# Attention of the last two batches inside the first MLP's first quads, on three PSUM banks, with two weight slots

## What is computed

```python
mask = np.abs(pos[:, None] - pos[None, :]) < factor        # factor = 4
out = sm_attn(q_d, k_d, v_d) repeated 4 times + masked attention of q, k, v
...
h = x @ w_in                   # 512 -> 2048
x = (h - np.tanh(h)) @ w_out   # 2048 -> 512
...
gate = 1.0 / (1.0 + np.exp(-(x @ w_gate)))   # 512 -> 1536
x = (gate * (x @ w_val)) @ w_out             # 1536 -> 512
```

## Time and profile before

| | us |
|---|---|
| median of 3 runs | 949.58 (945.84 to 951.64) |
| profiled execution | 949.2 |
| its span, first to last instruction | 947.1 |
| TensorE busy in the span | 901.8 (95%) |
| VectorE, ScalarE, GpSimd busy | 577.1, 387.3, 300.5 |

### The profile page before, as it was taken

The page is one execution under the profiler, slowest core; times in us unless marked ns, Lnnn a source line. Parts: engine busy times, 40 slices in busy tenths (PEclk is TensorE's granted clock), DMA queues, the critical chain, the costliest instruction groups (busy, mean ns, idle before and its releaser), DMA issues.

```text
span 947.1 us, 15642 instructions
## 1 busy us (share of the span) xinstructions
PE 901.8 (95%) x6056; PEld 844.4 (89%) x6056; DVE 577.1 (61%) x901; ACT 387.3 (41%) x750; POOL 300.5 (32%) x251
## 2 busy tenths in 40 slices
PE   7877787999999999999998999999999999999997
PEld 5766577989999999999998999999999999999996
DVE  8777745666876566866668555556544456544445
ACT  4765645443533234433334544444322234222221
POOL 5978677674102000111015555741200001000000
PEclk8898969999999999999999999999999999999999
DMA  9677628667746464645421567679775555575411
GB/s 259 170 217 218 168 77 306 222 237 261 275 153 227 147 228 151 221 158 211 165 92 45 217 262 279 274 292 365 282 285 208 217 214 214 212 279 201 199 45 67
DMA packets 46089, 197.01 MB, mean 208 GB/s; under 512 B 3936, under 2 KB 15552, under 8 KB 33216
## 3 DMA queue, kind: packets, MB, share of 16 engines
q1 hardware_dynamic: 41984, 166.66, 48.9%
q0 software_dynamic: 4032, 29.36, 8.3%
HBM read 139.90 MB, written 56.10 MB: 207 GB/s over the span
## 4 chain that ended last, share of the span: by engine, by line
PE 79%; POOL 9%; DVE 3%; DMA 3%; issue 3%; ACT 2%; SPq 0%; POOLq 0%; DVEq 0%; ACTq 0%
PE banks L787 43%; PE banks L855 18%; PE banks L971 16%; DMA v_four<-in_v_dram 2%; POOL v_four L554 1%; POOL win L595 1%; POOL prob L561 1%; POOL mid L601 1%; POOL v_down L558 1%; ACT win L1035 1%; PE banks L765 1%; DMA qk<-in_k_dram 1%; POOL prob_d L561 1%; DVE x_op L1297 1%; PE banks L742 0%
## 5 line engine op out<-in xcount | busy, mean ns | idle before, releaser
L787 PE MATMUL banks<-x_op,pair 128*128 128x384 f32 x1512 | 278.5, 336 | 1.7 <-DVE cg_sum L1457 1.7
L787 PEld LDWEIGHTS banks<-x_op,pair 128*128 128x128 f32 x1512 | 266.7, 189 | 9.7 <-DVE cg_sum L1457 2.1
L855 PE MATMUL banks<-g_parts,mid 128*128 128x384 f32 x1152 | 228.4, 337 | 7.3 <-DVE x_all L1377 5.3
L855 PEld LDWEIGHTS banks<-g_parts,mid 128*128 128x128 f32 x1152 | 203.0, 189 | 10.2 <-DVE x_all L1377 7.3
L787 PE MATMUL banks<-x_op,win 128*128 128x384 f32 x1008 | 206.7, 342 | 4.3 <-ACT c_sum L1071 4.3
L787 PEld LDWEIGHTS banks<-x_op,win 128*128 128x128 f32 x1008 | 182.3, 193 | 5.5 <-ACT c_sum L1071 3.8
L971 PE MATMUL banks<-wout,p_parts 128*128 128x512 f32 x648 | 163.6, 393 | 1.7 <-issue 1.7
L1377 DVE TENSOR_TENSOR x_all<-banks,x_all 128x384 f32<-128x384 f32 x168 | 93.0, 555 | 83.3 <-PE banks L855 82.9
L971 PEld LDWEIGHTS banks<-wout,p_parts 128*128 128x128 f32 x648 | 120.3, 188 | 22.6 <-issue 2.1
L1482 DVE TENSOR_TENSOR x_all<-banks,x_all 128x512 f32<-128x512 f32 x90 | 62.1, 690 | 113.4 <-PE banks L971 113.4
L617 POOL DMA_DIRECT2D wout<-kept_out x12 | 6.4, 537 | 211.4 <-PE banks L971 211.4
(11 more groups left out here) (93 smaller groups left out, 1008.8 us busy)
## 6 DMA issues: line engine op xcount, KB each, us to landing
pair<-kept_pair SPq DMA_DIRECT2D x24, 1792.0 KB, 10.8
win<-kept_in SPq DMA_DIRECT2D x16, 1792.0 KB, 7.4
kept_pair<-pair SPq DMA_DIRECT2D x12, 1792.0 KB, 11.8
mid<-kept_mid POOLq DMA_DIRECT2D x16, 1024.0 KB, 5.1
kept_in<-win SPq DMA_DIRECT2D x7, 1792.0 KB, 6.8
wout<-kept_out POOLq DMA_DIRECT2D x12, 1024.0 KB, 11.7
kept_mid<-mid SPq DMA_DIRECT2D x7, 1024.0 KB, 7.0
kept_out<-wout SPq DMA_DIRECT2D x6, 1024.0 KB, 14.6
```

The source lines that it names most:

```text
L787: mm = pe.matmul(bk[:, 0:T], weights[:, w, p - 1, kk, :], x_op[:, p - 1, x, kk, :], start=(first and kk == 0 and a == 0), stop=(last and k ...
L855: mm = pe.matmul(bk[:, 0:T], w[:, wp, f, m * P:(m + 1) * P], g[:, gp, 2 * f + t, :], start=(f == 0 and a == 0), stop=(f == 1 and a == 2))
```

## The change

Only units 0 to 9 (`SOLO`) are scored in the attention's own loop, and only units 0 to 7 (`EARLY`, those which the first 768 tokens need) pass it whole. Quad 0 follows unit 7. In quad n from 1 on, unit n+9 is scored (n up to 6), one head at a time in bank 3 (`head_scores`, `head_down_scores`); unit n+8 is normalised and turned in bank 4 (n up to 7); unit n+7 is multiplied with v in two parts in bank 5 (`first_values`, `second_values`, n up to 8). Those three banks were the second set of sums, so quads 0 to 8 all use banks 0 to 2: the first product of a quad now waits until all four g tiles of the quad before it are made. The weight slots of quads 0 to 7 go from three to two, for both weights, in the space that the attention's buffers leave; the third slot is used from quad 8 on. Raw weights of quad n+1 are asked for when the products of quad n-1 are done; their sums, high and low parts are made inside quad n. Quad 0 has another order of products and splits its x in halves. The raw w_out of the second MLP's first quad is loaded earlier. The core of the diff:

```diff
+FIRST_ORDER = (1, 2, 7, 6, 5, 4, 3)
+FIRST_SPLITS = ((1, None), (2, None), (5, None), (7, 0), (6, 0), (7, 1), (4, 0), (3, 0), (6, 1), (4, 1), (3, 1))
...
+    EARLY = PAIRS * -(-SUPER // S)
+    SOLO = EARLY + 2
...
-        MID = RING + 3 * WIN_BYTES
-        G = MID + 3 * MID_BYTES
+        MID = RING + 2 * WIN_BYTES
+        G = MID + 2 * MID_BYTES
...
+        MIXED = Q1 + 1
+        def sum_banks(n):
+            return B_SUM[n % 2 if n >= MIXED else 0]
...
+                if n >= 2:
+                    sp.wait_ge(s_p1, 7 * (n - 1))
+                    sp.wait_ge(s_kept[n % 2], kept_count(n - 2))
...
+            first_t1()
+            first_t2(0)
+            first_t4(0)
+            denominators(EARLY)
+            normalise(EARLY)
+            first_t2(1)
+            first_t4(1)
+            value_sums(EARLY)
             weight_low(1)
-            weight_sums(2)
...
-                    weight_sums(n + 2)
-                    weight_low(n + 2)
+            for n in range(1, N1):
+                t = EARLY + n
+                if t < UNITS:
+                    denominators(t)
+                    normalise(t)
                 if n + 1 < Q1:
-                    plain_low(n + 1)
-                if n % Q1 == 3:
+                    weight_sums(n + 1)
+                if 1 <= n - 1 < Q1:
+                    plain_low(n - 1)
+                if n + 1 < Q1:
+                    weight_low(n + 1)
+                if t < UNITS:
+                    value_sums(t)
+                if 4 <= n < 7:
...
+            def head_scores(u, hh):
+                slot, bk, head = ring3(u), bank[B_S], slice(hh * D, hh * D + D)
+                q_u, k_u = qk[slot][:, 0, :], qk[slot][:, 1, :]
+                if hh == 0:
+                    pe.wait_ge(s_qk[slot], 32 * uses(u, ring3))
+                    pe.wait_ge(s_exd, 4 * u)
+                else:
+                    pe.wait_ge(s_sub, scored(u, 0))
+                pe.matmul(bk[:, 0:HEAD], ident_b[:, :], mask_b[:, :, :].rearrange("p n c -> p (n c)"), start=True, stop=False,
+                          skip_group_check=True)
+                for w in range(NW):
+                    rows, col = slice(w % 2 * QW, w % 2 * QW + QW), w // 2 * KW
+                    mm = pe.matmul(bk[rows, col:col + KW], q_u[head, w * QW:(w + 1) * QW], k_u[head, FIRST_KEY[w]:FIRST_KEY[w] + KW],
+                                   start=False, stop=True, skip_group_check=True)
+                mm.then_inc(s_sl, 1)
+            def head_down_scores(u, hh):
...
-                    elif n == 1:
-                        pe.wait_ge(s_cr, 2 * UNITS)
+                        pe.wait_ge(s_sub, SOLO)
+                    elif n < MIXED:
+                        pe.wait_ge(s_g, 4 * n)
+                    elif n == MIXED:
+                        pe.wait_ge(s_x, valued(UNITS - 1))
                     else:
...
             def first_quad(n):
+                u, t, v = EARLY + n + 1, EARLY + n, EARLY + n - 1
+                if v < UNITS:
+                    first_values(v)
+                if u < UNITS:
+                    head_scores(u, 0)
                 first_product(n, 1)
                 next_block(n - 2, 4)
                 first_product(n, 7)
                 next_block(n - 2, 5)
+                if v < UNITS:
+                    second_values(v)
                 first_product(n, 6)
+                if u < UNITS:
+                    head_scores(u, 1)
                 next_block(n - 2, 6)
+                if t < UNITS:
+                    turn_local(t, 0)
                 first_product(n, 2)
                 next_block(n - 2, 7)
+                if t < UNITS:
+                    turn_rest(t, 0)
                 first_product(n, 5)
+                if u < UNITS:
+                    head_down_scores(u, 0)
                 next_block(n - 1, 0)
+                if t < UNITS:
+                    turn_local(t, 1)
                 first_product(n, 4)
                 next_block(n - 1, 1)
+                if t < UNITS:
+                    turn_rest(t, 1)
                 first_product(n, 3)
+                if u < UNITS:
+                    head_down_scores(u, 1)
                 next_block(n - 1, 2)
                 next_block(n - 1, 3)
...
+            values(EARLY - 1)
+            first_product(0, 1)
+            first_product(0, 2)
+            first_product(0, 7)
+            turn_local(EARLY, 0)
+            turn_local(EARLY, 1)
+            first_product(0, 6)
+            first_product(0, 5)
+            turn_rest(EARLY, 0)
+            turn_rest(EARLY, 1)
             first_product(0, 4)
             first_product(0, 3)
             for n in range(1, N1):
...
+            def head_exps(u, hh):
+                act.wait_ge(s_mxd, scored(u, hh))
+                act.wait_ge(s_exd, 4 * u)
+                act.activation(neg_max[0:HALF, 2 * hh:2 * hh + 2], row_max[0:HALF, 2 * (SLOTS + hh):2 * (SLOTS + hh) + 2], ACT.Copy,
+                               scale=-SCALE / FACTOR ** 2).then_inc(s_neg, 1)
+                if hh == 0:
+                    act.wait_ge(s_tr, 2 * (before(u, ring3) + 1))
+                    act.wait_ge(s_den, u)
+                act.wait_ge(s_neg, scored(u, hh))
+                for a in range(2):
+                    i = 2 * hh + a
+                    col = 2 * SLOTS + i
+                    act.activation(prob_d[ring3(u)][:, i, :], bank[B_S][0:HALF, a * SD:(a + 1) * SD], ACT.Exp, bias=neg_max[0:HALF, i:i + 1],
+                                   scale=SCALE / FACTOR ** 2, accum_out=row_sum[0:HALF, col:col + 1]).then_inc(s_exd, 1)
             def copy_local(u, hh):
...
                 last, s = n % Q1 == Q1 - 1, n // Q1 + 1
-                first = n % Q1 == 0 and n > 0
-                if n > 0:
-                    g_high(n - 1, 1)
-                if skip < 1:
-                    copy_c(n, C11)
+                first = n % Q1 == 0
+                u, t, v = EARLY + n + 1, EARLY + n, EARLY + n - 1
+                if v < UNITS:
+                    copy_down(v)
+                g_high(n - 1, 1)
+                copy_c(n, C11)
                 if last:
                     x_high(s, 1)
                 if first:
                     x_high(s - 1, 4)
-                if skip < 2:
-                    copy_c(n, C22)
+                if 1 <= n - 1 < Q1:
+                    plain_high(n - 1)
+                copy_c(n, C22)
                 if last:
                     x_high(s, 7)
                 if first:
...
                 copy_c(n, C21)
                 if last:
                     x_high(s, 6)
-                if 3 <= n + 2 < Q1:
-                    weight_high(n + 2)
+                if n + 1 < Q1:
+                    weight_high(n + 1)
+                if u < UNITS:
+                    exp_local(u)
+                if t < UNITS:
+                    copy_local(t, 0)
                 tanh(n, C11)
                 if last:
                     x_high(s, 2)
+                if t < UNITS:
+                    copy_rest(t, 0)
                 tanh(n, C22)
+                if u < UNITS:
+                    head_exps(u, 0)
                 g_high(n, 0)
                 if last:
                     x_high(s, 5)
+                if t < UNITS:
+                    copy_local(t, 1)
                 tanh(n, C21)
+                if t < UNITS:
+                    copy_rest(t, 1)
                 tanh(n, C12)
-                if n == 0:
-                    weight_high(2)
-                if n + 1 < Q1:
-                    plain_high(n + 1)
+                if u < UNITS:
+                    head_exps(u, 1)
                 if n == N1 - 1:
                     g_high(n, 1)
                     weight_high(Q1)
...
+            copy_rest(EARLY - 1, 0)
+            copy_rest(EARLY - 1, 1)
+            exp_local(EARLY + 1)
+            first_x_high(5, None)
+            copy_down(EARLY - 1)
+            first_x_high(7, 0)
+            down_bias(EARLY + 1)
+            exp_down(EARLY + 1)
+            copy_c(0, C11)
...
             def first_quad(n):
                 last, s = n % Q1 == Q1 - 1, n // Q1 + 1
-                first = n % Q1 == 0 and n > 0
+                first = n % Q1 == 0
+                u, t, v = EARLY + n + 1, EARLY + n, EARLY + n - 1
+                if v < UNITS:
+                    write_part(v, 0)
+                if u < UNITS:
+                    head_max(u, 0)
+                    head_shift(u, 0)
                 add_block(n - 2, 4)
                 g_low(n - 1, 1)
+                if t < UNITS:
+                    inverses(t)
                 add_block(n - 2, 5)
                 if last:
                     x_low(s, 1)
                 if first:
                     x_low(s - 1, 5)
+                if v < UNITS:
+                    write_part(v, 1)
+                if u < UNITS:
+                    averages(u)
                 add_block(n - 2, 6)
                 if last:
                     x_low(s, 7)
                 if first:
```

(28 more changed lines are left out.)

787 lines of the change are left out of this document (472 added, 315 removed).

## The result

The changed kernel takes 965.29 us (median of 4 runs, 964.59 to 966.16) against 948.71 (median of 4): a ratio of 1.0175, 95% interval 1.0141 to 1.0209, slower by some 16.6 us. Its profiled execution took 964.59, with a span of 962.8.

The account below looks back on a forecast made before the run. TensorE bounds from the third quad on, GpSimd's chain the attention before; 88.1 + 25.5 + 5 x 26.7 + 19.6 + 16.3 put quad 9 at 283.0, 9.7 later, so 949.2 becomes 958.9; range 939 to 976.

Parts of the forecast that it names:

- unit 7's denominators: End of GpSimd's sums for unit 7 in the early attention, forecast at 60.3 us against 60.14 before.
- A mixed quad at 26.7: Quads 2 to 6, products with woven-in attention: 26.7 us each from TensorE's work, two stops and lost clock; bounds 23.8 to 28.5.
- The stops: TensorE's two waits per mixed quad, at each head's turn_rest for ScalarE's copy_local: 2.4 and 1.8 us.
- The clock: Slow clock after a mixed quad's first stop, falling on block 0 and pushing the second chain by 0.9 us.
- The mechanism: Mixed quads: ScalarE waits in weight_high for GpSimd's sums; copy_local queues behind, TensorE stands 2.4 us; second wait 1.8 us.
- "No gain" up to unit 7: Early attention: fewer waits for raw v are eaten by quad 1's weights moved ahead; denominators at 60.3 against 60.14.
- its first landmark: Early attention: unit 0's denominators on GpSimd at 10.83 us, from which the turns to unit 7 were summed.
- Quad 0 at 88: Quad 1's first product, needing quad 0's four g tiles, starts at 88 us; no earlier than 84, 92 with late hand-overs.
- the wait of 4 us: Quad 0: TensorE stands 4 us before product 7, which waits for unit 9's exponentials and starts at 73.5.
- The exclusion of `x_low` by `weight_low(1)`: Rule that VectorE's two-SBUF-input instructions and GpSimd's exclude each other; weighed only for g_low, nothing in the sum.
- product 3's addition behind tanh: Quad 0: product 3 waits for an addition behind tanh, whose place is after copy_rest(8), at 84 us.
- Rival 1: Mixed quads: the chain through weight_high is hidden, 21.4 us a quad, 31 us less than forecast, 928; chance 0.10.

Follow-up runs that it names:

- the first three runs: Changed kernel with copy_local(t, 0) ahead of weight_high: 953.11 us; with copy_local(t, 1) ahead of head_exps and g_high: 955.01; with both moves: 943.73.
- the run that removed it: Changed kernel with a wait on GpSimd so weight_low(1) starts only after VectorE's low parts of the first block's x: 964.06 us, ratio 1.0167.

## Why the prediction was right, and which of its steps were not

The range, the side and even the size held (958.9 forecast, 965.3 measured), but partly because errors cancel. Step by step:

| | forecast | measured | off |
|---|---|---|---|
| unit 7's denominators | 60.3 | 63.39 | +3.1 |
| from there to quad 1's first product | 27.8 | 30.88 | +3.1 |
| quad 1 | 25.5 | 26.56 | +1.1 |
| quads 2 to 6 | 133.5 | 131.1 | -2.4 |
| quad 7 | 19.6 | 20.56 | +1.0 |
| quad 8 | 16.3 | 16.54 | +0.2 |
| quad 9's start | 283.0 | 289.01 | +6.0 |

- **A mixed quad at 26.7** measured 26.42, out of three terms that were each off. (The prediction adds them with 21.6 for TensorE's own work; by its own 21.4 the quad is 26.5. Its 3.95 for the inverse is more than the terms beside it give, 3.65 to 3.9, but the trace has 3.97.) TensorE's own work was put at 15.6 + 5.8 = 21.4 from a unit's 5.3 us and 0.5 for smaller groups; it is 23.4, since heads kept apart and nine separate groups of small matmuls cost 2.0 more. The stops were put at 2.4 + 1.8; they cost 1.5 each, because the copy came when forecast and TensorE came later. The clock was to cost 0.9 and cost nothing: stops of 1.32 us left it at 1.00, on the side of the 1.20 us stop of the earlier trace rows. It fell where stops were longer: in quad 1 after 3.88 us (0.87 over the quad), and in quad 0 after 3.96.
- **The mechanism** (ScalarE's copy queued behind `weight_high`, and behind `head_exps` and `g_high`) is shown by the first three runs: each move takes one stop and leaves the other.
- **"No gain" up to unit 7** should have read a loss. The sum counted GpSimd alone, with the others in step. Against its first landmark unit 0 was 0.8 late from the start; two waits for inverses took 0.62 and 0.69 instead of 0.36; v sums of 1.99 and 1.25 lay beside VectorE's x parts, and three low parts of 1.14 took 3.4 where 3.0 was forecast. That VectorE had two more instructions ahead of its row sums was not in it at all.
- **Quad 0 at 88.** Up to product 7 it held: the wait of 4 us (3.96) is there, 13.4 us after unit 7's denominators, 13.2 forecast. The second 3.1 us came behind it, and most of them before `weight_low(1)` began: product 5 started 22.6 us after the denominators, where the forecast has the copy that it waits for at 19.8. Two things ahead of product 5 stood in the sum at nothing, the wait of product 7's second half for its low part (1.72) and the half clock behind the 3.96 us stop, at which product 6 took 2.73. How the 2.7 us divide between them and the later x parts wasn't measured. The exclusion of `x_low` by `weight_low(1)` was also at nothing: the prediction weighed it only for the mixed quads' `g_low`, where nothing was right (`g_low` took 0.95). It is the most visible term and the smaller one, 0.6 us by the run that removed it, hidden for the rest by the next wait, which the prediction had named (product 3's addition behind tanh).
- **Rival 1** (stops hidden, 928) was mis-sized like the forecast: with the stops really gone the changed kernel is at 943.7, not 928, because 21.4 a quad wasn't to be had and quad 1 starts 6 us or more later.

## What to carry to other kernels

When work is woven into a loop, put each engine's small hand-over copies ahead of its long off-path steps: here two copies of 0.6 us queued behind steps whose results were needed only later cost more than the change lost, and with them moved it gains 0.6%. Cost woven-in matmuls by the form they have there (heads in turn or apart, in how many groups), not by the mean of the block they came from. Before pricing a step on the critical chain, look for the wait right behind it: 4 us on the chain were worth 0.6. And before crediting an edit with a shorter stop, compare the granted clock ahead of it: a stop also shrinks when the work before it runs slower.

## What the runs showed of the hardware

- A VectorE instruction with two SBUF inputs (384 elements, 0.54 us at its shortest) took 4.85 us beside one GpSimd instruction of 4.0, and 5.27 beside four of 1.1 issued back to back; with GpSimd's put behind them, five such took 5.18 instead of 9.15. Shorter pieces issued back to back didn't let VectorE in.
- A stop of TensorE cost about 0.2 us more than its row shows (1.5 against 1.32), and each group of small matmuls between 384-column ones about 0.16 beyond its own length (1.4 for nine).
- Stops of 1.32 us twice in 26 left the granted clock at 1.00; after one of 3.96 it was 0.50 for 10 us. After the stops of 2.26 and 1.07 us in quad 0 of one kernel it was 0.51 for 10 us; in a kernel with stops of 3.34, 1.72 and 0.94 it was 1.00 in the same stretch. The size of a stop alone doesn't tell.
